# The second pair's first mixing layer, divided by batch into five units and spread over 23 chunks of the layer that follows

## The reference

```
a, b = S1 @ x, S2 @ x;  phi(x) = outer(a, b)              # q and k, 64 features, 4 heads of 32
x   = (phi(q) @ (phi(k).T @ v)) / (phi(q) @ sum(phi(k)) + 1e-6)
u   = x + real(fft(fft(x, tokens), channels))             # mixed rows
un  = (u - mean(u)) / sqrt(var(u) + 1e-6)                 # over the 128 channels
x2  = u + relu(un @ w_ch1) @ w_ch2                        # layer 1, inner width 512
h   = relu(x2 @ w_in)                                     # layer 2, inner width 1024
gate = sigmoid(conv(h, 3 taps along the tokens))
out = (h * gate) @ w_out
```

## Time and profile before

| | kernel before |
|---|---|
| median of three runs | 285.07 us |
| the profiled execution | 284.65 us |
| its span | 282.8 us |
| PE busy | 256.7 us, 91% |
| DVE busy | 219.0 us, 77% |
| ACT busy | 187.3 us, 66% |
| POOL busy | 37.9 us, 13% |
| mean granted TensorE clock | 0.982 |

### The profile page before, as it was taken

The page is one execution under the profiler, slowest core; times in us unless marked ns, Lnnn a source line. Parts: engine busy times, 40 slices in busy tenths (PEclk is TensorE's granted clock), DMA queues, the critical chain, the costliest instruction groups (busy, mean ns, idle before and its releaser), DMA issues.

```text
span 282.8 us, 4304 instructions
## 1 busy us (share of the span) xinstructions
PE 256.7 (91%) x1524; PEld 214.3 (76%) x1524; DVE 219.0 (77%) x384; ACT 187.3 (66%) x353; POOL 37.9 (13%) x90
## 2 busy tenths in 40 slices
PE   8999999997999999797878589989999999999956
PEld 7999999897999888686656357767677787777623
DVE  0846869977877888628769737958599999999993
ACT  2432427235365666568599549777899899999933
POOL 0000000006033333215408600000000000000000
PEclk9999999999799999999999959999999999999999
DMA  6949510300000000000000000000100010001002
GB/s 206 386 164 414 172 71 0 90 1 2 0 0 3 0 1 2 1 2 1 0 0 0 2 0 0 0 3 0 73 6 2 0 79 0 1 3 79 0 0 79
DMA packets 4341, 13.04 MB, mean 46 GB/s; under 512 B 736, under 2 KB 1504, under 8 KB 4320
## 3 DMA queue, kind: packets, MB, share of 16 engines
q1 hardware_dynamic: 4320, 12.77, 12.4%
HBM read 10.54 MB, written 2.23 MB: 45 GB/s over the span
## 4 chain that ended last, share of the span: by engine, by line
DVE 25%; PE 15%; ACT 6%; POOL 4%; issue 1%; POOLq 0%; DVEq 0%
DVE arena L979 8%; DVE arena L972 8%; DVE arena L967 8%; PE ps L547 7%; PE ps L508 2%; PE ps L465 2%; ACT arena L758 2%; PE ps L466 2%; PE ps L467 1%; ACT arena L745 1%; ACT arena L670 1%; POOL arena L346 1%; PE ps L458 1%; ACT arena L753 1%; POOL arena L338 1%
## 5 line engine op out<-in xcount | busy, mean ns | idle before, releaser
L547 PE MATMUL ps<-arena,wout 128*128 128x364 f32 (+1 forms) x192 | 65.6, 481 | 3.5 <-DVE arena L979 3.3
L547 PEld LDWEIGHTS ps<-arena,wout 128*128 128x128 f32 x192 | 36.3, 194 | 22.2 <-DVE arena L979 5.8
L465 PE MATMUL ps<-x2hi,wlo 128*128 128x364 f32 x96 | 42.9, 447 | 11.1 <-ACT arena L745 11.0
L745 ACT ACTIVATE arena<-ps 128x364 f32<-128x364 f32 x96 | 40.8, 471 | 8.0 <-PE ps L467 7.8
L967 DVE SCALAR_TENSOR_TENSOR arena<-arena,taps 128x1088 f32<-128x1088 f32 x32 | 43.2, 1350 | 3.2 <-ACT arena L753 3.2
L979 DVE TENSOR_TENSOR arena<-arena 128x1088 f32<-128x1088 f32 (+2 forms) x36 | 41.5, 1166 | 4.2 <-ACT arena L758 4.2
L972 DVE SCALAR_TENSOR_TENSOR arena<-arena,taps 128x1088 f32<-128x1088 f32 x32 | 43.3, 1352 | 0.1
L753 ACT ACTIVATE arena<-arena,taps 128x1088 f32<-128x1088 f32 x32 | 38.5, 1203 | 1.0
L758 ACT ACTIVATE arena<-arena 128x1088 f32<-128x1088 f32 x32 | 35.3, 1102 | 4.6 <-DVE arena L972 4.6
L465 PEld LDWEIGHTS ps<-x2hi,wlo 128*128 128x128 f32 x96 | 18.1, 189 | 19.7 <-ACT arena L745 16.0
L467 PE MATMUL ps<-x2hi,whi 128*128 128x364 f32 x96 | 31.6, 330 | 0.0
(11 more groups left out here) (81 smaller groups left out, 458.9 us busy)
## 6 DMA issues: line engine op xcount, KB each, us to landing
arena<-v_d SPq DMA_DIRECT2D x4, 594.0 KB, 4.2
arena<-qT_d SPq DMA_DIRECT2D x3, 545.0 KB, 6.6
arena<-kT_d SPq DMA_DIRECT2D x3, 544.5 KB, 5.7
out_d<-arena SPq DMA_DIRECT2D x3, 544.0 KB, 2.7
cos_t<-cos_d SPq DMA_DIRECT2D x1, 926.5 KB, 5.7
sin_t<-sin_d SPq DMA_DIRECT2D x1, 926.5 KB, 7.5
arena<-qT_d SPq DMA_DIRECT2D x2, 272.5 KB, 4.4
wraw<-w_d SPq DMA_DIRECT2D x2, 256.0 KB, 5.3
```

Of the source, the lines that this page charges most:

```text
L465: pe.matmul(out, lo, rhi, start=first, stop=False)
L547: pe.matmul(ps[:, OUT_BANK + t, 0:z - a], wout[:, c, :], gate[:, i % GATES, a:z], start=(c == 0), stop=(c == C2 - 1)).then_inc(wout_done, 1)
L745: act.activation(h2[:, i % HIDDENS, t * TT:(t + 1) * TT], ps[:, bank_p(n), 0:TT], ACT.Relu).then_inc(h2_ready, 1)
```

## The change

The five rows of the second pair become five units that need not be one row of both batches. Unit 5 is batch 2, token tiles 0 and 1 of both halves; unit 6 is batch 2, tiles 2 and 3; unit 7 is tile 4 of batches 2 and 3; units 8 and 9 are batch 3. Units 0 to 4 are the rows of the first pair. So batch 2 is complete after unit 7, and layer 2 waits for the last unit of each batch (`LAST_UNIT`): chunk 16 for unit 7, chunk 24 for unit 9. `slots_before` follows a broken line (`PACES`): 23 slots ahead of layer 2, 11 more in its first 15 chunks, eight more in the next eight.

Since a unit needs up to four mixed rows, these no longer go to a ring of their own but are added in place in `x_nat`, and token sums, mixed rows and moments have tables that say in which slot they stand (`SUMS_AT`, `MIXED_AT`, `MOMENTS_AT`). The statistics are in rings of three. The hidden tiles have three banks (0, 3, 4) while there are slots. The transposes of un move from bank 0 to `up`'s bank 2 for units 6 to 9. `normed_transposes(0)` stands after the last piece of attention. `normed_low` is done in slot c = 2 from row 5 on.

```diff
-MIX_STEPS = 15
+UNITS = [[(side, b, r) for side in range(2) for b in range(BP)] for r in range(NJ)]
+for b_, j_ in ((2, 0), (2, 2), (2, 4), (3, 0), (3, 2)):
+    UNITS.append([(side, b_, j_ + k_) for side in range(2) for k_ in range(2)] if j_ < NJ - 1
+                 else [(side, b_ + k_, j_) for side in range(2) for k_ in range(2)])
+ROWS_OF = [1 + max((b // BP) * NJ + j for _, b, j in unit) for unit in UNITS]
+X2_WRITES = [3 if unit[0][1] == unit[1][1] else 2 for unit in UNITS]
+SUMS_AT = {3: 3, 7: 4, 9: 5, 11: 6, 13: 7, 15: 8, 18: 9}
+MIXED_AT = {0: 2, 4: 3, 8: 4, 10: 5, 12: 6, 14: 7, 16: 8, 19: 9}
+MOMENTS_AT = {1: 2, 5: 3, 9: 4, 13: 5, 17: 6, 20: 7, 22: 8, 25: 9}
+LAST_UNIT = {0: 4, 2 * C2: 7, 3 * C2: 9}
+PACES = ((0, 23), (30, 34), (46, 42))
...
         def bank_turned(r):
-            return 1 if r <= NJ else 0
+            return 1 if r <= NJ else 2
...
         def bank_p(n):
-            return 3 + n % 2 if n < NT * NI // 2 else (n - NT * NI // 2 + 3) % 5
+            return (0, 3, 4)[n % 3] if n < NT * MIXED_CHUNKS else (0, 3, 4, 1, 2)[(n - NT * MIXED_CHUNKS) % 5]
...
-        FIRST_SLOTS = NC1 // 2 + 4
-        ALL_SLOTS = NC1 + 2
+        FIRST_SLOTS = PACES[0][1]
+        MIXED_CHUNKS = PACES[-1][0] // 2
...
         def slots_before(place):
-            more = (ALL_SLOTS - FIRST_SLOTS) * place
-            return min(ALL_SLOTS, FIRST_SLOTS + -(-more // (2 * MIX_STEPS)))
+            for (p0, n0), (p1, n1) in zip(PACES, PACES[1:]):
+                if place <= p1:
+                    return n0 + -(-(n1 - n0) * (place - p0) // (p1 - p0))
+            return NC1 + 2
...
-                if c == 3 and r + 3 < NR:
-                    token_sums(r + 3)
+                if n in SUMS_AT:
+                    token_sums(SUMS_AT[n])
                 if c == 2 and r + 1 < NR:
                     normed_transposes(r + 1)
...
-                if i % (BP * C2) == 0 and t == 0:
-                    pe.wait_ge(x2hi_ready, 2 * NJ * (i // (BP * C2) + 1))
+                if i in LAST_UNIT and t == 0:
+                    pe.wait_ge(x2hi_ready, written(LAST_UNIT[i]))
...
             for n in range(len(AT_PIECES)):
                 attend(B - 1, n)
-                if n == 1:
-                    normed_transposes(0)
+            normed_transposes(0)
...
-                        dve.tensor_tensor(u[:, r % 4, side, :, half_ * 64:half_ * 64 + 64],
-                                          x_nat[:, q * BP:(q + 1) * BP, side * NJ + j, half_ * 64:half_ * 64 + 64],
-                                          spec[:, side ^ half_, :, half_:half_ + 64], ALU.add).then_inc(u_ready, 1)
+                        x = x_nat[:, q * BP:(q + 1) * BP, side * NJ + j, half_ * 64:half_ * 64 + 64]
+                        dve.tensor_tensor(x, x, spec[:, side ^ half_, :, half_:half_ + 64], ALU.add).then_inc(u_ready, 1)
...
                 if n < NC1 and has_low(n):
                     hidden_low(n)
-                if c == 0 and r + 2 < NR:
-                    mixed_rows(r + 2)
+                if n in MIXED_AT:
+                    mixed_rows(MIXED_AT[n])
                 if c == 1 and r >= NJ:
                     mixed_low(r - 1)
-                if c == 1 and r + 2 < NR:
-                    moments(r + 2)
+                if n in MOMENTS_AT:
+                    moments(MOMENTS_AT[n])
                 if c == 2 and 1 <= r < NJ:
                     mixed_low(r - 1)
-                if c == 3 and r + 1 < NR:
+                if c == (3 if r < NJ else 2) and r + 1 < NR:
                     normed_low(r + 1)
```

More of the change, by code:

```diff
@@ L160, in build @@
         negmean = room(TQ, 2 * BP)
-        rstd = room(TQ, 2, 2 * BP)
-        shift = room(TQ, 2, 2 * BP)
+        rstd = room(TQ, 3, 2 * BP)
+        shift = room(TQ, 3, 2 * BP)
         h1 = room(128, 3, G1)
@@ L251, in products, with written @@
             return i + 1 if i < SPLIT_FROM else SPLIT_FROM + NT * (i - SPLIT_FROM) + t + 1
+        def written(unit):
+            return sum(X2_WRITES[:unit + 1])
         def projected(i):
@@ L260, in slots_before, with normalised, token_views @@
         def slots_before(place):
-            more = (ALL_SLOTS - FIRST_SLOTS) * place
-            return min(ALL_SLOTS, FIRST_SLOTS + -(-more // (2 * MIX_STEPS)))
+            for (p0, n0), (p1, n1) in zip(PACES, PACES[1:]):
+                if place <= p1:
+                    return n0 + -(-(n1 - n0) * (place - p0) // (p1 - p0))
+            return NC1 + 2
+        def normalised(unit):
+            return [x_nat[:, b, side * NJ + j, :] for side, b, j in UNITS[unit]]
+        def token_views(x2, r):
+            for side in range(2):
+                turned = ps[:, bank_x2(r), side * BP * TQ:(side + 1) * BP * TQ]
+                (_, b0, j0), (_, b1, j1) = UNITS[r][side * BP:(side + 1) * BP]
+                if b0 != b1:
+                    rows, (_, columns) = token_range(j0, side)
+                    yield turned.rearrange("p (b t) -> p b t", t=TQ)[:, :, rows], x2[:, b0:b1 + 1, columns]
+                elif side == 1:
+                    for k in range(2):
+                        rows, (_, columns) = token_range(j0 + k, side)
+                        yield turned[:, k * TQ + rows.start:k * TQ + rows.stop], x2[:, b0, columns]
+                else:
+                    first, step = (1, 1) if j0 in LOW else (1 + S // 2, -1)
+                    yield (turned.rearrange("p (j t) -> p t j", t=TQ),
+                           x2[:, b0, first:first + step * 2 * TQ:step].rearrange("p (t j) -> p t j", j=2))
         def slots_a(i):
@@ L473, in normed_transposes @@
                 claim(bank, (unhi_ready, r + 1), (unlo_ready, r + 1))
-                for side in range(2):
-                    for b in range(BP):
-                        m = side * BP + b
-                        out = ps[:, bank, m * TQ:(m + 1) * TQ]
-                        mm = pe.transpose(out, un[:, side, b, :], ident[0:TQ, 0:TQ])
+                for m in range(2 * BP):
+                    mm = pe.transpose(ps[:, bank, m * TQ:(m + 1) * TQ], un[:, m, :], ident[0:TQ, 0:TQ])
                 mm.then_inc(ut_done, 1)
@@ L687, in mixed_high @@
                 act.wait_ge(w2_done, C1 * (r + 1))
-                for side in range(2):
-                    rows, columns = token_range(r, side)
-                    act.activation(x2hi[:, columns[0], columns[1]],
-                                   ps[:, bank_x2(r), side * BP * TQ:(side + 1) * BP * TQ].rearrange("p (b t) -> p b t", t=TQ)[:, :, rows],
-                                   ACT.Copy).then_inc(x2hi_ready, 1)
+                for turned, tokens in token_views(x2hi, r):
+                    act.activation(tokens, turned, ACT.Copy).then_inc(x2hi_ready, 1)
             def slot(n):
@@ L699, in slot @@
                     normed_rows(r + 1)
-                if c == 3 and r + 3 < NR:
-                    sine_copy(r + 3)
+                if n in SUMS_AT:
+                    sine_copy(SUMS_AT[n])
                 if c == 1 and r >= 1:
@@ L913, in mixed_low @@
             def mixed_low(r):
-                dve.wait_ge(x2hi_ready, 2 * (r + 1))
-                for side in range(2):
-                    rows, columns = token_range(r, side)
-                    dve.tensor_tensor(x2lo[:, columns[0], columns[1]],
-                                      ps[:, bank_x2(r), side * BP * TQ:(side + 1) * BP * TQ].rearrange("p (b t) -> p b t", t=TQ)[:, :, rows],
-                                      x2hi[:, columns[0], columns[1]].bitcast(F32), ALU.subtract).then_inc(x2lo_ready, 1)
+                dve.wait_ge(x2hi_ready, written(r))
+                for (turned, tokens), (_, high) in zip(token_views(x2lo, r), token_views(x2hi, r)):
+                    dve.tensor_tensor(tokens, turned, high.bitcast(F32), ALU.subtract).then_inc(x2lo_ready, 1)
             def slot(n):
```

47 lines of the change are left out of this document (23 added, 24 removed).

## The result

The changed kernel takes 275.38 us (median of 4 runs, 274.99 to 275.60), the kernel before, timed beside it on the same chip, 285.06 (4 runs, 284.86 to 285.19). The ratio is 0.966, 95% interval 0.965 to 0.968: faster by 9.7 us, where the forecast was 274.7 us in a range of 269.5 to 281.5.

A forecast was written before the change was run, and what follows sets the result against it. PE and DVE wait in turns from 130.3 to 205.8 us; DVE bounds afterwards. First tile 124.0, chunk 6 at 146.0, chunk 23 at 225.7, last left tap 260.4, span 272.4 with handovers: 274.7 us, range 269.5 to 281.5.

The forecast's parts named there:

- The last attention: Ahead of layer 2: eight matmuls fill PE's 1.56 us gap and avoid the slow clock behind it, -2.6 us.
- To the first tile: Ahead of layer 2: 122.03 - 2.6 + 2.5 - 1.2 + 2.7 + 0.6 puts PE's first tile at 124.0.
- The first left tap and chunks 0 to 5: Start of layer 2: first left tap at 129.2; DVE sets the pace, PE enters chunk 6 at 146.0.
- Rival 1: Chunks 1 to 5: clock falls where PE is busy some 60%; costs 3 us, 277.7; chance 0.17.
- Chunks 6 to 22: PE bounds: 4.66 us per slot chunk, 79.7 us in all, so chunk 23 starts at 225.7.
- what closes the loop is that a tile takes the bank of two before: Chunks 11 and 12 before the change: ring through ACT takes 5.38 us against PE's 4.66; third bank taken to break it.
- Rival 5: Slot chunks from 6 on: PE's third tile still waits for ACT, 5.38 for 4.66 us each; 289.3; chance 0.05.
- The pieces of x2: ACT's x2 copies in three pieces for one-batch units: 0.2 us each taken, hidden; exposed, 4 at most.
- To the end: From chunk 23: chunk 24 at 230.9, its tap at 234.3, then DVE bounds; chunk 31's tap 260.4, span 271.5.
- The 0.9 added for handovers: At the end of the sum: 0.9 us for handovers left out, making the span 272.4.
- Statistics: Sign to look for: no ACT wait for POOL after 130 us.
- The rule against it: Two-input VectorE and SBUF-reading GpSimd instructions block each other, so moved POOL chains could hold DVE up; changes no term.

The follow-up runs named there:

- the kernel with front and double projects together: Changed kernel with last mixed rows and unit 7's moments one slot later, double projects in chunks 24 and 28: 272.68 us, ratio 0.957.
- with eight slots: Changed kernel with all remaining 19 slots dealt evenly over the first 15 chunks, eight falling on chunks 0 to 5: 280.81 us, ratio 0.984.
- The late double projects: Changed kernel with the two chunks that project twice moved from 19 and 23 to 24 and 28: 274.60 us, ratio 0.963.
- the late run: Changed kernel with the last unit's moments in slot 29 instead of slot 25: 275.30 us, ratio 0.966.
- The square: Changed kernel with two or three hidden-tile banks, slots over 15 or 23 chunks: two banks 281.9 and 287.0 us, three banks 280.8 and 275.4.

## Why the prediction was right, step by step

**The last attention.** Predicted -2.6 with the clock; undoing it cost 3.1. Right, clock included, and 0.5 short.

**To the first tile.** Predicted 124.0, measured 123.06. 0.65 of the 0.9 is luck: the profiled execution was ahead of that of the kernel before by so much at PE's first transposes (12.81 for 13.46), where the change has no part. `up(20)` waited 2.58 for 2.7 predicted. That the clock could fall behind it (0.81 from 112 to 121 us) was not foreseen there. What the prediction gave as the whole cause, the mixed rows, was half: moving them left 1.25. The 1.5 us at `up(22)`, there when the clock holds, is no term of the sum.

**The first left tap and chunks 0 to 5.** 129.2 and 146.0 predicted, 128.46 and 145.89 measured. Rival 1 happened in small: PE stood 2.31 us at 137.33, and the stretch from 123.06 to 145.89 has 0.93. It cost nothing here. From first tile to first `project` this execution took 24.59 us; the kernel with front and double projects together, which has the same wait and a clock of 1.00 from 126 to 146 us, took 24.56. The sum hit the mark, but its picture, DVE's work and ACT's order, is only a part: the runs with two banks (4.5 us) and with eight slots (first `project` 159.80) show that banks and the density of slots bound them as well, of which the prediction says nothing.

**Chunks 6 to 22.** 4.66 a slot chunk predicted, 4.65 to 4.67 measured in chunks 15 to 18; chunk 23 at 225.7 predicted, 226.36 measured. ACT's output copy ahead of a relu of bank 2 was priced at 1.1 and made PE wait 1.23 at 190.24. The step "what closes the loop is that a tile takes the bank of two before" was right in direction and wrong in form: not 0.7 us in each slot chunk, but 1 to 2 us at a unit's end and in the first chunks. Rival 5 had 289.3 for it; with two banks it was 287.02.

**The pieces of x2.** ACT 0.66 to 0.67 and DVE 0.74 to 0.75 us for three; before, two pieces beside the chunks took 0.60 to 0.63 and 0.68. So some 0.05 a unit on each, under the 0.2 taken.

**To the end.** This is the term that was off. Chunk 24 was to start at 230.9 and its left tap, from which DVE bounds, to stand at 234.3, 3.4 us later. The start was 231.54, 0.6 late, but the tap came at 235.90, 4.4 later: it did not wait for chunk 24's tiles but for DVE's own work, which has no gap from x2 of unit 9 on (225.33). The handover to DVE is two to three chunks earlier than the prediction's, because DVE stood still 2.44 us for chunk 20 behind the double `project` of chunk 19, which the prediction had priced on PE alone (1.8), and again for x2, and owed its taps from there. Chunk 31's tap was at 262.00 for 260.4, 1.6 us late. PE's 0.6 can be in that only by way of unit 9's x2, the last thing that DVE waited for; how the 1.6 divide is not shown. The late double projects confirm the place and show that it is not all to be had: -0.8, since x2 holds DVE next. The 0.9 added for handovers covered half, and the span was 273.2 for 272.4. That the total came so near is in part luck: 0.9 us too early at the first tile, 1.6 too late at the last tap, and 0.9 added without a place.

**Statistics.** No wait of ACT for POOL after 130 us, as said. That taking them sooner matters was never a term, and the late run shows that it does not.

**The rule against it.** While unit 9's chain ran on POOL, DVE took 3.70 us from one left tap to the next (137.80 to 141.50). POOL's first operation there took 1.21 us and its second 1.96, where unit 8's, with no tap beside them, took 0.20 and 1.04. The trace again shows only one of the two held up.

Two sums of the rivals are off by a little: 274.7 + 7 is 281.7, not 281.5, and 14 x 0.72 is 10.1, not 9.9. Nothing rests on them.

What the forecast did not say is that its parts don't add. It took the bank as a condition and spreading as the gain, and rival 5 had the kernel slower without the condition, as it was. The square says more: each is worth its full gain only with the other.

## What to carry to other kernels

Price a buffer and a schedule together: the third PSUM bank brought 1 to 4 us in one order of work and 11.6 in another, and the order lost 5.1 without it. A buffer taken from one use is paid by the next: whenever two things share a bank, look where the slower of its readers stands in its engine's program (one line moved gave 9.4 us, another bank for two units 3.3). A wait removed can come back at the next consumer: x2 behind the double projects, 0.79 to 2.01 us, and the slot behind the first tiles, 0.45 to 1.63. So follow the engine that bounds, here to its first left tap, and stop only when that moves. But compare with an execution at the same clock before you say that a wait has moved: the one at `up(22)` had only been hidden.
